# A mixture-of-experts kernel on one core: the dense second layer as seven products of sums (Strassen) over two token tiles

## What is computed

```python
# 1. linear attention with exp features, 8 heads of 64 -> x (2304 x 512)
# 2. dense mixture: every token through all 8 experts
logits = x @ w_gate; P = exp(logits - logits.max())
for _ in range(8):
    P /= P.sum(1, keepdims=True) + 1e-09
    P /= P.sum(0, keepdims=True) + 1e-09
    P *= N / E
for e in range(8):
    h = np.maximum(x @ w1[e], 0.0)         # 512 -> 1024
    out += P[:, e:e + 1] * (h @ w2[e])     # 1024 -> 512
# 3. routed mixture: every token through one expert, that of the largest logit
expert_idx = argmax(normed(out) @ normed(expert_emb).T / tau)
y[mask] = gate_w[mask, None] * (np.maximum(x[mask] @ w1b[e], 0.0) @ w2b[e])
```

## Time and profile before

| | us |
|---|---|
| median of three runs | 2100.82 (2100.05 to 2101.99) |
| profiled execution, its own time | 2100.28 |
| its span, first to last instruction | 2098.5 |
| TensorE busy | 2035.2 |
| VectorE busy | 1018.8 |
| ScalarE busy | 686.6 |
| GpSimd busy | 179.1 |

### The profile page before, as it was taken

The page is one execution under the profiler, slowest core; times in us unless marked ns, Lnnn a source line. Parts: engine busy times, 40 slices in busy tenths (PEclk is TensorE's granted clock), DMA queues, the critical chain, the costliest instruction groups (busy, mean ns, idle before and its releaser), DMA issues.

```text
span 2098.5 us, 31563 instructions
## 1 busy us (share of the span) xinstructions
PE 2035.2 (97%) x12600; PEld 1211.0 (58%) x12600; DVE 1018.8 (49%) x1614; ACT 686.6 (33%) x1354; POOL 179.1 (9%) x183
## 2 busy tenths in 40 slices
PE   6999899999999999999999999999999999599998
PEld 5788655555555555555555555555555565377775
DVE  7888755544444444444444444444444424434343
ACT  3566443323323333232233332232333322122221
POOL 0553400000000000000000000000000000111110
PEclk9999999999999999999999999999999999699999
DMA  6233111121122112312211221221122221831600
GB/s 200 63 69 68 47 41 41 72 104 67 41 81 81 41 41 91 111 41 81 82 41 41 81 93 66 84 81 41 41 81 81 81 106 41 335 131 44 266 27 8
DMA packets 93103, 169.38 MB, mean 81 GB/s; under 512 B 60438, under 2 KB 60566, under 8 KB 89760
## 3 DMA queue, kind: packets, MB, share of 16 engines
q1 hardware_dynamic: 88960, 157.92, 21.4%
q0 software_dynamic: 4000, 9.45, 1.3%
HBM read 126.19 MB, written 44.83 MB: 81 GB/s over the span
## 4 chain that ended last, share of the span: by engine, by line
PE 94%; DMA 2%; DVE 2%; issue 0%; SPq 0%; POOL 0%; ACT 0%; POOLq 0%; DVEq 0%
PE ps L635 35%; PE ps L652 35%; PE ps L819 6%; PE ps L803 4%; PE ps L584 3%; PE ps L597 3%; PE ps L805 2%; DMA arena<-split_weights 2%; PE ps L563 2%; PE ps L572 1%; PE ps L550 1%; PE ps L692 1%; PE ps L776 0%; DMA tau_sb<-in_moe_tau_dram 0%; DVE vmp L1134 0%
## 5 line engine op out<-in xcount | busy, mean ns | idle before, releaser
L635 PE MATMUL ps<-arena 128*128 128x384 f16 x4608 | 775.9, 326 | 3.8 <-ACT arena L918 3.4
L652 PE MATMUL ps<-arena 128*128 128x512 f16 x3456 | 770.7, 379 | 0.0
L635 PEld LDWEIGHTS ps<-arena 128*128 128x128 f16 x4608 | 450.8, 98 | 316.5 <-ACT arena L918 3.8
L652 PEld LDWEIGHTS ps<-arena 128*128 128x128 f16 x3456 | 338.6, 98 | 392.2 <-issue 1.7
L914 ACT ACTIVATE arena<-ps 128x384 f32<-128x384 f32 x384 | 188.5, 491 | 1029.7 <-PE ps L635 1017.0
L1194 DVE TENSOR_TENSOR arena<-arena 128x384 f16<-128x384 f32 x384 | 214.1, 558 | 318.5 <-ACT arena L918 317.3
L1249 DVE SCALAR_TENSOR_TENSOR arena<-ps,wt,arena 128x512 f32<-128x512 f32 x126 | 94.6, 751 | 436.4 <-PE ps L652 436.3
L918 ACT ACTIVATE arena<-ps 128x384 f16<-128x384 f32 x384 | 185.9, 484 | 0.0
L1085 DVE TENSOR_REDUCE wg<-arena 128x1 f32<-128x1024 f32 x128 | 154.9, 1211 | 28.7 <-DMA arena<-in_moe_w_dram 28.6
L1101 DVE SCALAR_TENSOR_TENSOR arena<-arena,wsc 128x1024 f16<-128x1024 f32 x124 | 158.4, 1278 | 0.8 <-ACT arena L888 0.6
L803 PE MATMUL ps<-arena 128*128 128x256 f16 x800 | 139.2, 278 | 5.3 <-issue 3.4
...
## 6 DMA issues: line engine op xcount, KB each, us to landing
...
```

What stands on the lines that cost most here:

```text
L635: last = pe.matmul(o, ring[:, slot, sw, FF * c + 128 * j:FF * c + 128 * j + 128], xT[:, sx, c, BLK * blk:BLK * blk + BLK], start=(n == 0), ...
L652: last = pe.matmul(ps[:, Y_PS + tt, :], hbuf[:, blk % 2, sh, f, 128 * tt:128 * tt + 128], ring[:, slot, 2 + sw, D * f:D * f + D], start=(n ...
```

## The change

The second layer of the dense mixture is computed for two token tiles at a time. With the hidden values split in four quarters (two tiles, two halves of the contraction) and the weights in four (two halves of the contraction, two of the columns), seven products of a quarter or a sum of quarters give the four quarters of the output (Winograd's form of Strassen's scheme). A product is 12 matmuls of 256 columns. Blocks are of 256 tokens, so there are 9 an expert and 72 slots; the hidden units are 12 matmuls of 256 columns. VectorE makes four sums of hidden values for each two units; ScalarE and VectorE cut three values and four sums to halves. Two chains of products run in two PSUM regions (one of them double, banks 4 and 5); after each product VectorE adds the region's present state to one quarter of the accumulator. Scaling, sums and low halves of the second layer's weights are GpSimd's, the high halves ScalarE's; the seven operands go out to DRAM and come back by ScalarE's DMA queue once the product that used the buffer has ended. The tables PLANS say for each kind of expert which weight step stands behind which quarter block (h = 4 x block + quarter). Expert 0's second weights are made on GpSimd between the last pairs of the attention; one buffer of cut_x is dropped, and the attention's loop is written out. In the routing, 12 tiles are early instead of 15, the table's six columns are made and multiplied in two halves, with the late rows' gates between, and the load of stage 3's expert 0 comes before the stores of the rows; that of expert 2 waits for the third gather.

```diff
-BLK = 384
+BLK = 256
...
+Q = FC // 2
+OPS = 7
+HC = D // 2
+DONE = OPS * NB
+UNIT = tuple(p + Q * x for p in range(Q) for x in range(2))
...
+        A11, A12, A22, S1, S2, S3, S4 = range(OPS)
+        PRODUCT = (A11, A12, S2, S1, S3, S4, A22)
+        INTO = (0, 1, 0, 1, 0, 1, 0)
+        RESULT = ((0, 0), (0, 0), (0, 1), (1, 1), (1, 1), (0, 1), (1, 0))
+        FRESH = (0, 2, 3, 6)
+        PIECES = (A11, A12, S4, S1, S3, S2, A22)
+        PIECES0 = (A11, A12, S4, S2, S1, S3, A22)
...
+        def source(buf, o):
+            q11, q12, q21, q22 = quarters(buf)
+            return {A11: q11, A12: q21, S4: q22, S1: q11, S3: q12, S2: q22, A22: q21}[o]
...
+        def region(n, u):
+            return ps[:, 6 if n else 4 + u, 0:HC]
...
+            "rest": dict(
+                order=("S", "B0", "B1", "A"), staged=MIXED,
+                top={0: ("S", 0), 1: ("S", 2), 2: ("B0", 0), 4: ("B0", 2), 17: ("B1", 0), 18: ("B1", 2), 20: ("A", 0), 21: ("A", 2)},
+                scale={3: "S", 7: "B0", 21: "B1", 24: "A"},
+                hi={6: (("S", 0),), 8: (("B0", 0), ("S", 1)), 10: (("B0", 1), ("S", 2)), 12: (("B0", 2), ("S", 3)),
+                    14: (("B0", 3), ("S", 4)), 17: (("S", 5), ("S", 6)), 21: (("B1", 0),), 22: (("B1", 1),), 24: (("B1", 2),),
+                    25: (("B1", 3),), 27: (("A", 0), ("A", 1)), 28: (("A", 2), ("A", 3))},
+                lo={9: (("B0", 0),), 11: (("B0", 1),), 13: (("B0", 2),), 15: (("B0", 3),), 22: (("B1", 0),), 23: (("B1", 1),),
+                    25: (("B1", 2),), 26: (("B1", 3),), 28: (("A", 0), ("A", 1)), 29: (("A", 2), ("A", 3))}),
...
+            def both_parts(i):
+                o = PIECES0[i]
+                pool.tensor_copy(w2op[:, o, 0], source(raw, o)).then_inc(w2hi_done, 1)
+                pool.wait_ge(w2hi_done, i + 1)
+                pool.tensor_tensor(w2op[:, o, 1], source(raw, o), w2op[:, o, 0], ALU.subtract).then_inc(w2lo_done, 1)
+
+            def first_second_weights(i):
+                q11, q12, q21, q22 = quarters(raw)
+                if i == 9:
+                    across(wm[:, 1, :], wg[:, 1, :], RMAX, wmax_done, 2, wall_done)
+                if i == 10:
+                    scaled(8, 0, q11, 0)
+                    scaled(8, 1, q12, 0)
+                if i == 11:
+                    pool.wait_ge(w2sc_done, 1)
+                    both_parts(0)
+                    summed(-1, 0, raw, 1)
+                if i == 12:
+                    scaled(8, 2, q21, 0)
+                    pool.wait_ge(w2sc_done, 3)
+                    both_parts(1)
+                if i == 13:
+                    scaled(8, 3, q22, 0)
+                    pool.wait_ge(w2sc_done, 4)
+                    both_parts(2)
+                if i == 14:
+                    summed(-1, 1, raw, 3)
+                    summed(-1, 2, raw, 3)
+                if i == 15:
+                    pool.wait_ge(w2sum_done, 3)
+                    for k in (3, 4, 5):
+                        both_parts(k)
+                    summed(-1, 3, raw, 3)
+                    pool.wait_ge(w2sum_done, 4)
+                    both_parts(6)
                     if i in SPLIT:
                         split_weights(0, SPLIT[i])
+                    first_second_weights(i)
...
+                    if plan == "rest":
+                        top_of("S")
+                        top_of("B0")
+                        scale(0, q11)
+                        scale(1, q12)
+                        low(0)
+                        summed(e, 0, buf, 1)
+                        scale(2, q21)
+                        low(1)
+                        scale(3, q22)
+                        low(2)
+                        for k in range(1, 4):
+                            summed(e, k, buf, 3)
+                        for k in range(3, OPS):
+                            low(k)
+                        top_of("B1")
+                        top_of("A")
...
+            def product(e, blk, ub, k, u):
+                o, n = PRODUCT[k], INTO[k]
+                if blk == 0:
+                    if isinstance(e, int) and e == 0:
+                        pe.wait_ge(w2lo_done, PIECES0.index(o) + 1)
+                    else:
+                        pe.wait_ge(w2op_in[o], 16 * e)
+                if k == 0:
+                    pe.wait_ge(hlo_done, FC * (ub + 1) - 1)
+                if k == 2:
                     pe.wait_ge(hlo_done, FC * (ub + 1))
+                free = OPS * ub + {0: 0, 1: 6 - OPS, 2: 1, 3: 2, 4: 3, 5: 4, 6: 5}[k]
+                if due(free):
+                    pe.wait_ge(yacc_done, free)
+                i = 0
+                for p in range(Q):
                     for sh, sw in ((0, 0), (0, 1), (1, 0)):
+                        last = pe.matmul(region(n, u), hop[:, u, sh, p, o, :], w2op[:, o, sw, p, :],
+                                         start=(i == 0 and k in (0, 1, 3)), stop=(i == 3 * Q - 1), skip_group_check=True)
+                        i += 1
...
+                        for k in range(OPS):
+                            product(e, blk, ub, k, (par + blk) % 2)
+                            if end:
+                                last_rows(k)
+                            for n in range(2 * k, 2 * k + 2 if k < Q and not end else 2 * k):
+                                if blk < NB - 1:
+                                    hidden(e, blk + 1, ub + 1, n, par)
+                                else:
+                                    hidden(e + 1, 0, ub + 1, n, 1 - par)
+                                if last and par == 1:
+                                    rows_between(blk, n)
...
+            def relu_rows(ub, blk, n):
+                p, x = divmod(n, 2)
+                act.wait_ge(h1_done, FC * ub + n + 1)
+                if x == 0 and due(FC * ub + n - 2):
+                    act.wait_ge(hlo_done, FC * ub + n - 2)
+                dst = tb[:, p % 2, 1:3, :] if x else tb[:, p % 2, 0:S3 + 1:S3, :]
+                act.activation(dst, hidden_ps(blk, n).rearrange("p (r n) -> p r n", r=2), ACT.Relu,
+                               scale=2.0 ** -HDOWN).then_inc(hrelu_done, 1)
+
+            def operands_hi(ub, u, p):
+                act.wait_ge(hrelu_done, FC * ub + 2 * p + 2)
+                if p == 0 and due(OPS * (ub - 1)):
+                    act.wait_ge(y_done, OPS * (ub - 1))
+                act.activation(hop[:, u, 0, p, 0:3, :], tb[:, p % 2, 0:3, :], ACT.Copy).then_inc(hhi_done, 1)
+                act.wait_ge(hsum_done, 4 * (Q * ub + p + 1))
+                act.activation(hop[:, u, 0, p, 3:OPS, :], tb[:, p % 2, 3:OPS, :], ACT.Copy).then_inc(hhi_done, 1)
...
+            def operand_sums(ub, p):
+                t = tb[:, p % 2]
+                base = 4 * (Q * ub + p)
+                dve.wait_ge(hrelu_done, FC * ub + 2 * p + 2)
+                dve.tensor_tensor(t[:, S1, :], t[:, S3, :], t[:, A22, :], ALU.add).then_inc(hsum_done, 1)
+                dve.wait_ge(hsum_done, base + 1)
+                dve.tensor_tensor(t[:, S3, :], t[:, A11, :], t[:, S3, :], ALU.subtract).then_inc(hsum_done, 1)
+                dve.tensor_tensor(t[:, S2, :], t[:, S1, :], t[:, A11, :], ALU.subtract).then_inc(hsum_done, 1)
+                dve.wait_ge(hsum_done, base + 3)
+                dve.tensor_tensor(t[:, S4, :], t[:, A12, :], t[:, S2, :], ALU.subtract).then_inc(hsum_done, 1)
+            def operands_lo(ub, u, p, x):
+                some = slice(0, 3) if x == 0 else slice(3, OPS)
+                dve.wait_ge(hhi_done, FC * ub + 2 * p + x + 1)
+                if x == 1:
+                    dve.wait_ge(hsum_done, 4 * (Q * ub + p + 1))
+                dve.tensor_tensor(hop[:, u, 1, p, some, :], tb[:, p % 2, some, :], hop[:, u, 0, p, some, :], ALU.subtract)\
                    .then_inc(hlo_done, 1)
...
+            def accumulate(e, blk, ub, k, plan, u):
+                r, d = RESULT[k]
+                j = BT * blk + r
+                dst, src = acc[:, j, HC * d:HC * d + HC], region(INTO[k], u)
...
+                    dve.wait_ge(y_done, OPS * ub + k + 1)
+                    by = wt[:, j:j + 1]
+                if k not in FRESH:
+                    dve.wait_ge(yacc_done, OPS * ub + k)
+                dve.scalar_tensor_tensor(out=dst, in0=src, scalar=by, in1=dst, op0=ALU.mult, op1=ALU.add)\
+                   .then_inc(yacc_done, 1)
...
+                        for p in range(Q):
+                            weights_hook(plan, c, par, e, Q * blk + p)
...
+                            operand_sums(ub + 1, p)
+                            operands_lo(ub + 1, 1 - u, p, 0)
+                            accumulate(e, blk, ub, p + 1, plan, u)
+                            operands_lo(ub + 1, 1 - u, p, 1)
+                        for k in (5, 6):
+                            accumulate(e, blk, ub, k, plan, u)
...
+            def columns(c0, c1):
+                shape = [128, NT, c1 - c0, MT]
+                dve.tensor_tensor(sels[:, :, c0:c1, :], ohs.unsqueeze(2).broadcast_to(shape),
```

(5 more changed lines are left out.)

830 lines of the change are left out of this document (509 added, 321 removed), and 3 rows, old and new, of the table hi.

## The result

The changed kernel takes 2346.4 us (median of 4 runs, 2341.33 to 2348.98) against 2101.21 us for the kernel before (4 runs): a ratio of 1.117, 95% interval 1.115 to 1.118. Forecast were 2124 us, in a range of 2078 to 2172. The direction was right, the size wrong by 222 us, and the range didn't hold it. The profiled execution of the changed kernel has a span of 2344.5 us and a mean granted clock of 0.951, where that of before had 2098.5 and 0.986.

What follows compares the result with a forecast made beforehand. TensorE, busy 97% of the span, was taken as the bound. From 2100.3 us, -79.9 + 57.5 + 5.8 + 38 + 7.6 - 5 = +24.0 gave 2124.3 us, 1.1% slower, range 2078 to 2172.

Steps and rivals of the forecast that it cites:

- Matmuls, -79.9: Dense layers on TensorE: all matmuls 256 columns wide at 109.2 ns, fewer in the second layer, saving 79.9 us.
- Product 0's wait, +57.5: Block boundaries: TensorE waits 0.81 us for the last accumulation of the block before, 71 times, adding 57.5 us.
- ScalarE and GpSimd ... hidden by TensorE: Dense part: ScalarE has room and GpSimd's 36 us an expert run in its own queue, costing nothing.
- The forecast's own sign of being wrong: Listed signs against the forecast: a 19.7 us period, sums over 0.33 us beside GpSimd, or TensorE waiting for DMA or ScalarE.
- Rival 2: Dense part: VectorE becomes the bound, its two-SBUF-operand work and GpSimd excluding each other, +47 us to 2171 us; chance 0.16.
- VectorE late through weight work, +38: Dense blocks: weight work on VectorE exceeds a quarter block's free time and delays TensorE, 38 us, bounds 0 to 85.
- 5.8 in all: Product 6 in each block needs accumulation 4, which VectorE reaches 0.08 us late at best; 72 times, +5.8 us.
- The start, +7.6: End of attention: GpSimd's first weight sums between the last pairs delay the dense part by 7.6 us, bounds 0 to 12.
- The tail, -5: From last output to routing table, VectorE's chain gets shorter by 5 us, bounds -8 to +2.
- Rival 1: Dense part: VectorE is never late, weight work falls into gaps and the 38 us go, 2086 us; chance 0.14.
- Rival 3: Dense second layer: products are as many as outputs, nothing is saved and 2200 us result; chance nearly nil.

Runs made afterwards that it cites:

- run 2: The changed kernel with product 0 no longer waiting for the last accumulation of the block before: 2308.54 us.
- run 7: run 4 with the eighth hidden unit moved behind product 4 and accumulation 4 ahead of the last pair's sums on VectorE: 2074.84 us.
- run 4: The changed kernel with the edits of run 1, run 2 and run 3 together, GpSimd's values left out: 2124.64 us.
- run 1: The changed kernel with GpSimd's scalings, sums and low halves of second-layer weights cut to 8 columns in the dense part, values left out: 2200.98 us.
- run 9: run 10 with GpSimd's second-layer weight work in the attention begun one pair earlier, nothing behind pair 14; computes everything: 2061.2 us.
- run 6: The changed kernel with the edits of run 2 and run 3, dense second-layer weight work moved from GpSimd to VectorE and ScalarE; computes everything: 2192.84 us.
- run 5: A separate kernel timing six VectorE operations of a kind alone and beside four GpSimd operations; beside GpSimd's subtraction, held ones grew by 6.06 to 6.20 us.
- run 10: run 6 plus the order of run 7, with weight work of experts 2 to 6 dealt out one piece a slot, but for two pairs of maxima: 2064.78 us.
- run 3: The changed kernel with SyncE's wait and the second-layer weight load moved from behind attention pair 6 to behind pair 8, their maxima later too: 2318.34 us.

## Why the prediction was wrong

**Matmuls, -79.9: right at the full clock.** The quiet block of 20.48 us becomes 19.72 with product 0 free (run 2) and 19.65, the forecast's figure, with the new order (run 7). So the two waits of a quiet block are 0.76 and 0.07 us, where 0.81 and 0.08 were forecast. What the sum lacks is that matmuls behind long waits run at the lower clock: some 48 us in the dense part, 3 before.

**Product 0's wait, +57.5: right for each boundary, too large in the sum.** Released with GpSimd silent it gave back 48.3 us (the remainder of run 4), in the changed kernel 37.9 (run 2). Where VectorE is late anyway, the boundary's 0.8 us are part of a longer wait.

**"ScalarE and GpSimd ... hidden by TensorE": the step that failed.** GpSimd's 36 us an expert were priced at nothing, and they cost 145.4 us (run 1). I had asked whether anybody waits for GpSimd's results; the question is also whom GpSimd keeps from working while it runs. The forecast's own sign of being wrong, sums over 0.33 us while GpSimd works, is there: 2.38 at 1686.13. Rival 2 named the mechanism. Its rule is that of the Trainium skill, and it had a chance of 0.16 since I held that no row of before shows such a pair. In dense work that is so: GpSimd is idle there. But the attention has one, in the timeline of before:

```profile
252.78 1.14 DVE L1149 TENSOR_TENSOR gsc<-gsc,xsc 128x1 f32<-128x1 f32 x1
```

It multiplies two single columns in SBUF. It began under GpSimd's L465, which ran from 252.50 to 253.90, and ended at 253.92. In run 9 the same operation began under a scaling of GpSimd and took 0.16 us. So the trace of before did speak for this rival, in one row: 1.14 us for a product of two columns was a price to ask about.

Its size failed as well: 254 x 37% = 94 us of overlap, half on the path, 47. Measured: 136.3 us of VectorE's time, 113.6 us of waits ahead of the products and 31.2 us of slower matmuls behind them. The overlap of two busy shares is the wrong sum for a lock. 70 of GpSimd's 77 low halves and sums met a VectorE operation that they held, and it lost the rest of GpSimd's, up to 2.1 us for an operation of 0.29; and the half on the path came from a VectorE with slack, where runs 6 and 4 show 70% of added work in the time even without a lock.

The Trainium skill, SBUF - State Buffer, "SBUF: two separate sides", says that the shared port pair is an exclusive lock which whoever starts first keeps for the whole instruction, and that VectorE takes it with two SBUF inputs or in a 2-port mode. The rows agree: 2.38 us for 0.29 at 1686.13, 1.28 us kept at 1682.68, and the copy and column scaling of run 5. GpSimd's scaling doesn't agree: in run 5 it lasted 2.84 us or more, and the six sums beside it grew by 0.80 us in all. I had drawn on another page of the Trainium skill and sized the rule by overlapping time.

**VectorE late through weight work, +38: right in kind, too small.** (The sum of 5 x 4.8 and 14.4 leaves out the last expert's 1 us.) In run 1, without the lock, experts 0 to 6 take 1360 us over 63 blocks; at 20.48 they would take 1290. That is 70 us where some 37 of the 38 were meant. Queues were laid out by hand, and two things were missed. Accumulation 4 sits behind the last sums, and the eighth hidden unit runs behind product 3 already (run 7: 49.8 us for both), which I had priced at 0.08 us a block, 5.8 in all, as the best case. And lumps of two pieces exceed a slot (run 10: 43.7 us, with the added work of run 6).

**The start, +7.6: wrong by some 43 us.** The first product begins at 323.45 us; before, the first output began at 277.75. Eight units of 256 columns are 96 x 53.3 ns = 5.1 us shorter than eight of 384, so the forecast's first product was at 280.2. 28.1 us are SyncE's queue (run 3). The forecast spoke of the maxima that move into the attention and called them hidden; the load in front of them, and its wait, move too, and pairs 7 to 15 of q, k and v stand behind it. Some 6 us more lie in the pair from 213.44 us on, which takes 19.8 us where the one ahead took 13.7: in it VectorE waits 5.66 us for GpSimd's all-reduce, itself 6.70 us late for nothing that the profile shows (below). This is read from the trace, no run takes it away. Run 9, with less GpSimd work between the first hidden unit and the first product, brings 5.6 us back there. The rest I haven't taken apart.

**The tail, -5: right.** From the last output or product to the end it was 321.8 us (2098.5 less 1776.7) and is 316.4 (2344.5 less 2028.1).

Together: 2124.3 + 145.4 for the lock and the clock behind it + 28.1 for SyncE's queue + 33 for VectorE's lateness + 15 for the rest of the start is 2346, against 2346.4. The first two are measured by runs of their own, the last two are remainders read from traces, so that it closes this well proves nothing about them. Rival 1 wanted a VectorE that is never late: only the new order and the dealt-out work come near it (run 9, 18.4 us of waits ahead of the products). Rival 3 never arose: L950 has its 6048 matmuls.
